# Attention and two channel mixers on one core: loads of both heads merged, and the load of grouped values moved from SyncE's queue to GpSimd's

## The chip, the cores and the metric

The kernel runs on one core of a Trainium2 chip. The metric is device time in microseconds (us) for one execution. Before the change three executions took 503.38, 504.46 and 505.86 us, so the median is 504.46 us. A core has a matrix engine (TensorE, PE), a vector engine (VectorE, DVE), a scalar engine (ScalarE, ACT), GpSimd (POOL) and SyncE (SP). Each runs its own instructions in order and they meet at semaphores. Loads from device memory go through 16 DMA engines.

## The reference

For batch 2, 8 heads, 768 positions and head dimension 64, every query attends to the keys less than 16 positions away and to 24 summaries, one per block of 32 positions: the maximum of the block's keys, with the mean of its values. Two channel mixers follow.

```python
k_sum = k.reshape(B, H, nb, 32, D).max(axis=3)
v_sum = v.reshape(B, H, nb, 32, D).mean(axis=3)
scores_l = where(|i - j| < 16, scale * q @ k.T, -1e9)
scores_s = scale * q @ k_sum.T + log(32)
a = softmax(concat([scores_l, scores_s], -1))
x = a @ concat([v, v_sum])                      # then heads side by side: (2, 768, 512)
h = relu(x.T @ w_tok1) @ w_tok2;  u = x + h.T   # mixing over positions
y = u + relu(u @ w_ch1) @ w_ch2                 # mixing over channels
# second mixer: xk, xr mix y with y shifted by one position
out = sigmoid(xr @ w_r) * (relu(xk @ w_k) ** 2 @ w_v)
```

## The kernel before

Attention works on pairs of heads: 16 (batch, head) rows make 8 pairs, p = 0 to 7. Pairs 0 to 5 are a loop of three turns with two pairs each (par is 0 or 1 and picks one of two buffers), pairs 6 and 7 stand behind it. A pair has three groups (r = 0, 1, 2) of four units, a unit being 64 queries of both heads. While pair p is computed, pair p+2 is prepared, with its own loads:

- kn and qn are the keys and queries as they lie in memory, turned by the PE (line 895), copied by ACT and DVE into kt and qbd.
- v8 holds the values of both heads in rows of 8 positions (96 rows, 2 heads, 512 values). POOL's `sum_values` adds them in three steps, v8 to v4 (line 436), v4 to v2 (438), v2 to v1 (441). The PE then sums groups of four rows of v1 into the 24 block means (`sum_vs`, line 918), ACT writes them to vsb, and SP spreads vsb over the twelve units of vw (`spread_vs`, line 321).
- vw holds the windows of values that the PE multiplies with the turned weights aT (line 998). For each head there are ten windows of 96 rows in the middle and one of 80 rows at each end.

No scheduler moves anything: every engine runs what is written, in that order. What matters here is the order of four of them within pair p.

**PE**, `pair`: for each r it turns the exponentials (line 976), forms scores of pair p+1 (928), and multiplies by the values (998). In r = 0 it turns kn of pair p+2 between scores and values, in r = 1 qn. In r = 2 `sum_vs(p + 2)` stands between scores and values, and it waits for v1 of pair p+2.

**POOL**, `pair`: `sum_values(p + 2)`, then the low part of a token-mixing weight (wt1L or wt2L, line 451), which waits for DVE's high part (733), then `split_x(p)` (line 457), which waits for the high part of the output of pair p itself (ACT, and DVE's line 724, after the last product of the pair and its normalisation). So POOL leaves pair p only after the PE has finished it.

**DVE**, after the values of r = 2: row sums (703), the weight's high part (733), the inverse (707), normalisation (716), high part of x (724).

**SP**, `pair`: spread vsb, four loads of kn and qn of pair p+2, a wait for `tree_step` and two loads of v8 of pair p+2, a wait until the PE has finished pair p-1 (`av_done`), six loads of vw of pair p+1, and one weight load into stg. v8 has one buffer; `tree_step` counts POOL's first two additions, so the load of pair p+2 may start once v4 of pair p+1 is there.

Ahead of the loop POOL fills constants (lines 400 to 431) and runs `sum_values(0)` and `sum_values(1)`. Semaphores that count loads go up by 16 for each.

Of the kernel before, what the change touches and what calls it, by code (L numbers as in the profile page):

```python
# [18 lines left out]
def build_program(nc, q, k, v, w_tok1, w_tok2, w_ch1, w_ch2, mu_k, mu_r, w_k, w_v, w_r, out):  # L19
    B, NH, S, D = q.shape  # L20
# [5 lines left out]
    SUMB, WIN = 32, 16  # L26
# [3 lines left out]
    UQ = 64  # L30
# [22 lines left out]
    with ctx:  # L53
# [159 lines left out]

        heads = "b h (t p j) d -> (b h) p t (j d)"
        q_rows = q.rearrange(heads, t=NB, j=2)
        k_rows = k.rearrange(heads, t=NB, j=2)
        v_rows8 = v.rearrange("b h (p j) d -> (b h) p (j d)", j=8)
        vt = v.tensor
# [4 lines left out]

        v_first = v_window(0, LOC - WIN, 1)
        v_mid = v_window(UQ - WIN, LOC, NU - 2)
        v_last = v_window(S - UQ - WIN, LOC - WIN, 1)
        w1_cols = w_ch1.rearrange("(k p) n -> p k n", p=P)
# [69 lines left out]
        def _(sp):  # L297
            def load_qk(p, par):
                for dst, src, loaded in ((kn, k_rows, ld_k), (qn, q_rows, ld_q)):
                    for h in range(2):  # L300
                        sp.dma_start(dst[par][:, h, :, :],  # L301
                                     src[bass.ds(2 * p + h, 1)].rearrange("o p t n -> (o p) t n")
                                     ).then_inc(loaded[par], 16)

            def load_vw(p, par):
                for h in range(2):
                    for dst, src in ((vw[par][WIN:LOC, 0:1, h, 0:D], v_first),
                                     (vw[par][0:LOC, 1:NU - 1, h, 0:D], v_mid),
                                     (vw[par][0:LOC - WIN, NU - 1:NU, h, 0:D], v_last)):
                        sp.dma_start(dst, src[bass.ds(2 * p + h, 1)].rearrange("o p t n -> (o p) t n")  # L310
                                     ).then_inc(ld_vw[par], 16)

            def load_v8(p):
                for h in range(2):
                    sp.dma_start(v8[:, h, :, :].rearrange("p j d -> p (j d)"),
                                 v_rows8[bass.ds(2 * p + h, 1)].rearrange("o p n -> (o p) n")
                                 ).then_inc(ld_v8, 16)

# [8 lines left out]
            load_qk(1, 1)  # L327
            load_v8(0)
            sp.wait_ge(init_pool, 2)
            load_vw(0, 0)  # L330
            with nc.allow_non_contiguous_dma(reason="two short vectors"):
                for n in range(2):
                    sp.dma_start(mu[:, n, :], mu_cols[n]).then_inc(ld_mu, 16)
            sp.wait_ge(tree_step, 1)
            load_v8(1)

            def pair(p, par, i=None):
                sp.wait_ge(qbank_read, 5 * p + 5)
                spread_vs(par)
                if i is not None:  # L340
                    sp.wait_ge(q_turned, 2 * p + 2)
                    sp.wait_ge(k_turned, 2 * p + 2)
                    load_qk(p + 2, par)
                    sp.wait_ge(tree_step, 2 * p + 3)
                    load_v8(p + 2)
                sp.wait_ge(av_done, 3 * p + 1)
                load_vw(p + 1, 1 - par)
                if i is not None:
                    sp.wait_ge(wl_done, p + 1)
                    src = t1_rows[:, bass.ds(2 * i, 2), :] if par == 0 else t2_rows[:, :, bass.ds(TOK * i, TOK)]  # L350
                    sp.dma_start(halves(stg[par][:, 0:512]), src).then_inc(ld_w[par], 16)
# [39 lines left out]
        def _(pool):  # L391
            steps = [0]

            def then(ins):
# [26 lines left out]
            for h in range(2):  # L421
# [9 lines left out]
                               pattern=[[-1, LOC]], channel_multiplier=0).then_inc(init_pool, 1)  # L431

            def sum_values(p):

                pool.wait_ge(ld_v8, 32 * p + 32)
                pool.tensor_tensor(v4[:, :, :, :], v8[:, :, 0:4, :], v8[:, :, 4:8, :], ALU.add).then_inc(tree_step, 1)
# [6 lines left out]
            def pair(p, par, i=None):  # L443
                if i is not None:
                    sum_values(p + 2)
                    pool.wait_ge(wh_done, p + 1)
# [12 lines left out]

            sum_values(0)  # L460
            sum_values(1)
            with pool.Fori(0, NP // 2 - 1) as i:
# [429 lines left out]
        def _(pe):  # L892
# [39 lines left out]
            pe.wait_ge(init_pool, 3)  # L932
            turn_k(0, 0, 32, None)
            turn_q(0, 0, 32, bT, False)
            pe.wait_ge(kt_written, 4)
            scores(0, 0, 0, 0, None)
            scores(0, 0, 1, 1, None)
            sum_vs(0, None)
            turn_k(1, 1, 32, 5)
            scores(0, 0, 2, 0, GU)  # L940
            turn_q(1, 1, 32)
            sum_vs(1, 7)
# [28 lines left out]
            def pair(p, par, prep):  # L971
                for r in range(NG):
# [7 lines left out]
                    if prep and r == 0:  # L980
                        turn_k(p + 2, par, 16 * (p - par) + 64, 5 * (p + 2))
                    if prep and r == 1:
                        turn_q(p + 2, par, 16 * (p - par) + 64)
                    if prep and r == NG - 1:
# [5 lines left out]
                    if r == 0:  # L990
                        pe.wait_ge(ld_vw[par], 48 * (p - par) + 96)
                        pe.wait_ge(ld_vs[par], 8 * (p - par) + 16)
# [152 lines left out]
```

## Time and profile before

| | |
|---|---|
| executions | 503.38, 504.46, 505.86 us; median 504.46 |
| span of the profiled execution | 501.4 us |
| PE busy over the span | 478.4 us (95%) |
| ACT busy / DVE busy / POOL busy | 191.6 / 221.7 / 114.6 us |
| instructions | 8399 |
| packets moved by DMA | 48657, 31.70 MB |

The profile is of one execution whose own total time is not given beside its span; the median of the executions is 3.1 us above that span. Busy time counts work on an engine, not waits. Attention fills the first 98 us; the rest is the mixers, in which the PE is nearly always busy. "SPq" or "POOLq" rows are an engine's queue at work on DMA issues or registers.

### The profile page before, as it was taken

How to read it: one execution, taken by the hardware profiler on the slowest of the kernel's cores; microseconds unless marked ns; L12 is line 12 of the kernel's file. 1: busy time of each engine (PE TensorE's matmuls, PEld its weight loads, DVE VectorE, ACT ScalarE, POOL GpSimd, SP SyncE). 2: the span in 40 equal slices, each digit the busy share in tenths (PEclk: the TensorE clock that was granted, in tenths of full speed). 3: DMA queues.
4: the chain of work that ended last, by engine and by line, in shares of the span. 5: the costliest groups of instructions: out<-in, count | busy, mean ns of one | idle time of the engine just before them, and what ended most of it. 6: DMA issues, size and time to landing. Idle time of an engine off the chain costs nothing.

```text
span 501.4 us, 8399 instructions
## 1 busy us (share of the span) xinstructions
PE 478.4 (95%) x2968; PEld 444.9 (89%) x2968; DVE 221.7 (44%) x575; ACT 191.6 (38%) x424; POOL 114.6 (23%) x98
## 2 busy tenths in 40 slices
PE   4798789998999999999999999999999999999996
PEld 4677678787999999999999999999889989989985
DVE  5598887499411141114111411456436355444521
ACT  3799887424211121112111211345455256353411
POOL 6364553285999000000000024300000000000000
PEclk9999999999999999999999999999999999999999
DMA  9999997144443100000000010000010001001001
GB/s 196 181 208 215 228 213 186 46 126 129 166 149 145 43 1 0 0 0 0 0 0 0 0 42 0 0 1 0 1 49 14 0 21 42 0 0 63 0 0 63
DMA packets 48657, 31.70 MB, mean 63 GB/s; under 512 B 21248, under 2 KB 42496, under 8 KB 48640
## 3 DMA queue, kind: packets, MB, share of 16 engines
q1 hardware_dynamic: 48640, 31.49, 26.4%
q8 instruction: 9, 0.15, 0.1%
q14 instruction: 8, 0.07, 0.1%
HBM read 27.14 MB, written 3.15 MB: 60 GB/s over the span
## 4 chain that ended last, share of the span: by engine, by line
PE 84%; SPq 5%; DMA 5%; ACT 2%; issue 2%; DVE 1%; POOL 0%; ACTq 0%; POOLq 0%
PE bank L946 26%; PE bank L947 26%; PE bank L948 26%; DMA kn<-in_k_dram 4%; SPq L301 2%; PE bank L998 1%; SPq L310 1%; DMA v<-in_v_dram 1%; PE bank L976 1%; ACT e_sb L518 1%; PE bank L1017 1%; ACT qbd L498 1%; PE bank L895 1%; SPq L321 1%; PE bank L928 1%
## 5 line engine op out<-in xcount | busy, mean ns | idle before, releaser
L845 DVE SCALAR_TENSOR_TENSOR rL<-bank,rH 128x384 fp32r<-128x384 f32 x48 | 26.7, 557 | 148.2 <-ACT rH L614 148.2
L614 ACT ACTIVATE rH<-bank 128x384 fp32r<-128x384 f32 x48 | 23.6, 492 | 163.1 <-PE bank L948 158.7
L946 PE MATMUL bank<-uH,W1H 128*128 128x384 f32 x192 | 64.8, 337 | 0.0
L947 PE MATMUL bank<-uL,W1H 128*128 128x384 f32 x192 | 64.6, 336 | 0.0
L948 PE MATMUL bank<-uH,W1L 128*128 128x384 f32 x192 | 64.4, 336 | 0.0
L947 PE MATMUL bank<-xkL,WkH 128*128 128x384 f32 x128 | 43.3, 338 | 0.0
L946 PE MATMUL bank<-xkH,WkH 128*128 128x384 f32 x128 | 43.1, 337 | 0.0
L948 PE MATMUL bank<-xkH,WkL 128*128 128x384 f32 x128 | 42.8, 335 | 0.0
L947 PEld LDWEIGHTS bank<-uL,W1H 128*128 128x128 f32 x192 | 36.1, 188 | 0.0
L948 PEld LDWEIGHTS bank<-uH,W1L 128*128 128x128 f32 x192 | 36.0, 188 | 0.0
L946 PEld LDWEIGHTS bank<-uH,W1H 128*128 128x128 f32 x192 | 36.0, 188 | 0.0
L482 POOL CAST W2aH<-stg 128x1024 fp32r<-128x1024 f32 x3 | 3.1, 1040 | 142.3 <-PE bank L948 142.3
L871 DVE SCALAR_TENSOR_TENSOR k<-bank,kr 128x384 f32<-128x384 f32 x32 | 17.8, 556 | 38.7 <-ACT kr L631 38.6
L948 PE MATMUL bank<-rH,W2aL 128*128 128x384 f32 x96 | 32.3, 336 | 0.0
L948 PE MATMUL bank<-rH,W2bL 128*128 128x384 f32 x96 | 32.3, 336 | 0.0
L946 PE MATMUL bank<-rH,W2bH 128*128 128x384 f32 x96 | 32.2, 335 | 0.0
L947 PE MATMUL bank<-rL,W2bH 128*128 128x384 f32 x96 | 32.2, 335 | 0.0
L946 PE MATMUL bank<-rH,W2aH 128*128 128x384 f32 x96 | 32.2, 335 | 0.0
L947 PE MATMUL bank<-rL,W2aH 128*128 128x384 f32 x96 | 32.2, 335 | 0.0
L631 ACT ACTIVATE kr<-bank 128x384 f32<-128x384 f32 x32 | 15.7, 489 | 43.1 <-PE bank L948 42.7
L518 ACT ACTIVATE e_sb<-s_sb,nmx 128x120 f32<-128x120 f32 x96 | 29.7, 382 | 3.3 <-DVE nmx L693 3.3
L928 PE MATMUL bank<-kw,qbd 128*128 128x120 f32 x192 | 27.6, 292 | 1.8 <-ACT qbd L498 1.6
(131 smaller groups left out, 1093.2 us busy)
## 6 DMA issues: line engine op xcount, KB each, us to landing
stg<-in_moe_w_ch_dram SPq DMA_DIRECT2D x12, 512.0 KB, 3.6
vw<-in_v_dram SPq DMA_DIRECT2D x16, 240.0 KB, 4.9
kn<-in_k_dram SPq DMA_DIRECT2D x16, 192.0 KB, 3.8
qn<-in_q_dram SPq DMA_DIRECT2D x16, 192.0 KB, 4.4
v<-in_v_dram SPq DMA_DIRECT2D x16, 192.0 KB, 5.1
out_dram<-o_sb SPq DMA_DIRECT2D x12, 256.0 KB, 2.0
stg<-in_moe_w_k_dram SPq DMA_DIRECT2D x4, 512.0 KB, 3.5
stg<-in_moe_w_v_dram SPq DMA_DIRECT2D x4, 512.0 KB, 3.4
```

Source lines behind the costliest of these rows:

```text
L301: sp.dma_start(dst[par][:, h, :, :], src[bass.ds(2 * p + h, 1)].rearrange("o p t n -> (o p) t n")).then_inc(loaded[par], 16)
L310: sp.dma_start(dst, src[bass.ds(2 * p + h, 1)].rearrange("o p t n -> (o p) t n")).then_inc(ld_vw[par], 16)
L321: sp.dma_start(vw[par][LOC:COLS, :, :, :].rearrange("p t h n -> p t (h n)"), vsb[par][:, :, :].rearrange("p h n -> p (h n)").unsqueeze(1) ...
L518: act.activation(e_sb[par][:, n, :], s_sb[r][:, n, :], ACT.Exp, bias=nmx[:, r, n:n + 1], scale=-1.0).then_inc(exp_done, 1)
L614: act.activation(rH[f % 2][:, :], bank[f % 2][:, 0:GR], ACT.Relu).then_inc(rh_done, 1)
L631: act.activation(kr[f % 2][:, :], bank[f % 2][:, 0:GR], ACT.Relu).then_inc(kr_done, 1)
L845: dve.scalar_tensor_tensor(out=rL[f % 2][:, :], in0=bank[f % 2][:, 0:GR], scalar=0.0, in1=rH[f % 2][:, :].bitcast(F32), op0=ALU.max, op1=A ...
L871: dve.scalar_tensor_tensor(out=k2[f % 2][:, :], in0=bank[f % 2][:, 0:GR], scalar=0.0, in1=kr[f % 2][:, :], op0=ALU.max, op1=ALU.mult).then ...
L928: ins = pe.matmul(bS[gp][:, COLS * n:COLS * n + COLS], qbd[par][:, t, :], kw[par][:, t, :], start=True, stop=True)
L946: pe.matmul(dst, wH, mH, start=start, stop=False, **more)
L947: pe.matmul(dst, wH, mL, start=False, stop=False, **more)
L948: return pe.matmul(dst, wL, mH, start=False, stop=stop, **more)
```

## The change

The loads of kn and of qn take both heads in one DMA each (six blocks of 128 values in place of three, twice). The end windows of vw take both heads in one DMA each, while the middle windows stay one per head. The load of v8 takes both heads in one DMA and is issued by POOL: for pair 0 as POOL's first instruction, for pair 1 between `sum_values(0)` and `sum_values(1)`, and for pair p+2 at the beginning of POOL's `pair`, just before `sum_values(p + 2)`. The semaphore counts follow. Bytes, packets and the arithmetic are the same. With spread and weight load, SP issues eight DMAs for a pair where it issued fourteen; POOL issues one.

```diff
             def load_qk(p, par):
                 for dst, src, loaded in ((kn, k_rows, ld_k), (qn, q_rows, ld_q)):
-                    for h in range(2):
-                        sp.dma_start(dst[par][:, h, :, :],
-                                     src[bass.ds(2 * p + h, 1)].rearrange("o p t n -> (o p) t n")
-                                     ).then_inc(loaded[par], 16)
+                    sp.dma_start(dst[par][:, :, :, :].rearrange("p h t n -> p (h t) n"),
+                                 src[:, bass.ds(2 * NB * p, 2 * NB), :]).then_inc(loaded[par], 16)
 
             def load_vw(p, par):
                 for h in range(2):
-                    for dst, src in ((vw[par][WIN:LOC, 0:1, h, 0:D], v_first),
-                                     (vw[par][0:LOC, 1:NU - 1, h, 0:D], v_mid),
-                                     (vw[par][0:LOC - WIN, NU - 1:NU, h, 0:D], v_last)):
-                        sp.dma_start(dst, src[bass.ds(2 * p + h, 1)].rearrange("o p t n -> (o p) t n")
-                                     ).then_inc(ld_vw[par], 16)
-
-            def load_v8(p):
-                for h in range(2):
-                    sp.dma_start(v8[:, h, :, :].rearrange("p j d -> p (j d)"),
-                                 v_rows8[bass.ds(2 * p + h, 1)].rearrange("o p n -> (o p) n")
-                                 ).then_inc(ld_v8, 16)
+                    sp.dma_start(vw[par][0:LOC, 1:NU - 1, h, 0:D],
+                                 v_mid[bass.ds(2 * p + h, 1)].rearrange("o p t n -> (o p) t n")
+                                 ).then_inc(ld_vw[par], 16)
+                for dst, src in ((vw[par][WIN:LOC, 0, :, 0:D], v_first),
+                                 (vw[par][0:LOC - WIN, NU - 1, :, 0:D], v_last)):
+                    sp.dma_start(dst, src[:, bass.ds(2 * p, 2), :]).then_inc(ld_vw[par], 16)
...
                     load_qk(p + 2, par)
-                    sp.wait_ge(tree_step, 2 * p + 3)
-                    load_v8(p + 2)
                 sp.wait_ge(av_done, 3 * p + 1)
...
         def _(pool):
             steps = [0]
+            pool.dma_start(v8[:, :, :, :].rearrange("p h j d -> p h (j d)"),
+                           v_rows8[:, 0:2, :]).then_inc(ld_v8, 16)
...
+            def load_v8(p):
+                pool.dma_start(v8[:, :, :, :].rearrange("p h j d -> p h (j d)"),
+                               v_rows8[:, bass.ds(2 * p, 2), :]).then_inc(ld_v8, 16)
+
             def sum_values(p):
 
-                pool.wait_ge(ld_v8, 32 * p + 32)
+                pool.wait_ge(ld_v8, 16 * p + 16)
...
             def pair(p, par, i=None):
                 if i is not None:
+                    pool.wait_ge(tree_step, 2 * p + 3)
+                    load_v8(p + 2)
                     sum_values(p + 2)
...
             sum_values(0)
+            pool.wait_ge(tree_step, 1)
+            load_v8(1)
             sum_values(1)
```

What POOL's queue holds in the loop, from one `split_x` (xL) to the additions of the next pair, first before, then with the change (each with the line numbers of its own kernel; v_79 is v8, v_80 is v4, v_81 is v2, v_82 is v1; ISA and REGISTER_ALU are address arithmetic and waits).

```order
L457 TENSOR_TENSOR xL<-u,xH 128x768
L435 ISA
L436 TENSOR_TENSOR v_80<-v_79 96x512 [waits ld_v8]
L437 ISA
L438 TENSOR_TENSOR v_81<-v_80 96x256 [waits tree_step]
```

```order
L456 TENSOR_TENSOR xL<-u,xH 128x768
L442 ISA
L427 ISA [waits tree_step]
L427 DMA v_79<-in_v_dram 96x2x512
L432 ISA
L433 TENSOR_TENSOR v_80<-v_79 96x512 [waits ld_v8]
```

The load now stands between the xL of one pair and the addition that reads what it loads.

SP's queue in the loop, from the wait for the finished pair to the last load of vw, first before, then with the change, where the row of qn just ahead is shown too (vw_73 is the buffer of odd pairs).

```order
L310 ISA [waits av_done]
L310 DMA vw_73<-in_v_dram 80x64
L310 ISA
L310 DMA vw_73<-in_v_dram 96x10x64
L310 ISA
L310 DMA vw_73<-in_v_dram 80x64
L310 ISA
L310 DMA vw_73<-in_v_dram 80x64
L310 ISA
L310 DMA vw_73<-in_v_dram 96x10x64
L310 ISA
L310 DMA vw_73<-in_v_dram 80x64
```

```order
L303 DMA qn_75<-in_q_dram 128x6x128
L337 ISA
L308 ISA [waits av_done]
L308 DMA vw_73<-in_v_dram 96x10x64
L308 ISA
L308 DMA vw_73<-in_v_dram 96x10x64
L313 REGISTER_ALU
L313 DMA vw_73<-in_v_dram 80x2x64
L313 ISA
L313 DMA vw_73<-in_v_dram 80x2x64
```

Two end loads are gone from this stretch, the two middle ones come first, and no load of v8 stands ahead of the wait.

## Rows read from the trace of the kernel before

**Rows 1.** The page: chain that ended last, by engine and by line.

```profile
PE 84%; SPq 5%; DMA 5%; ACT 2%; issue 2%; DVE 1%; POOL 0%; ACTq 0%; POOLq 0%
PE bank L946 26%; PE bank L947 26%; PE bank L948 26%; DMA kn<-in_k_dram 4%; SPq L301 2%; PE bank L998 1%; SPq L310 1%; DMA v<-in_v_dram 1%; PE bank L976 1%; ACT e_sb L518 1%; PE bank L1017 1%; ACT qbd L498 1%; PE bank L895 1%; SPq L321 1%; PE bank L928 1%
```

**Rows 2.** Busy time by stretch: start:end and length, engines, clock, DMA share, GB/s.

```profile
core 0: us, PE busy (x) PEld busy (x) DVE busy (x) ACT busy (x) POOL busy (x), PEclk, DMA share, GB/s
13.00:16.00 3.00, 1.51 (x7) 0.89 (x7) 0.90 (x8) 1.97 (x8) 1.09 (x2) 1.00 0.71 143
29.51:78.87 49.36, 42.81 (x491) 36.29 (x492) 42.03 (x201) 44.64 (x122) 27.80 (x25) 1.00 1.18 214
```

**Rows 3.** Timeline of SP's queue: start us, us, what; first loads, then one pair.

```profile
12.87 0.80 SPq L315 DMA_DIRECT2D v<-in_v_dram  x2
...
18.86 0.82 SPq L315 DMA_DIRECT2D v<-in_v_dram  x2
...
55.77 0.84 SPq L321 DMA_DIRECT2D vw<-vsb  x1
56.99 1.13 SPq L301 DMA_DIRECT2D kn<-in_k_dram  x2
58.22 0.97 SPq L301 DMA_DIRECT2D qn<-in_q_dram  x2
59.37 0.82 SPq L315 DMA_DIRECT2D v<-in_v_dram  x2
60.49 3.59 SPq L310 DMA_DIRECT2D vw<-in_v_dram  x6
64.27 0.39 SPq L351 DMA_DIRECT2D stg<-in_moe_w_tok_dram  x1
```

**Rows 4.** Timeline of the PE: last product of pairs 0, 3 and 5, and what precedes it.

```profile
14.22 0.62 PE L918 MATMUL bank<-v,sel 96*24 96x128 f32 x2 [1.04 <-POOL v L441]
...
28.77 0.74 PE L998 MATMUL bank<-vw,aT 120*64 120x65 f32 x16
...
58.59 0.40 PE L918 MATMUL bank<-v,sel 96*24 96x128 f32 x2 [0.80 <-POOL v L441]
58.91 0.74 PE L998 MATMUL bank<-vw,aT 120*64 120x65 f32 x16
...
78.14 0.73 PE L998 MATMUL bank<-vw,aT 120*64 120x65 f32 x16
```

**Rows 5.** Timeline of POOL: additions of pairs 0 to 2, then the turn of pair 3 to 4.

```profile
8.90 0.27 POOL L430 TENSOR_SCALAR_AFFINE_SELECT mask<-mask 128x96 f32<-128x96 f32 x1
11.57 1.27 POOL L436 TENSOR_TENSOR v<-v 96x512 f32<-96x512 f32 x1 [2.40 <-DMA v<-in_v_dram]
...
16.28 1.27 POOL L436 TENSOR_TENSOR v<-v 96x512 f32<-96x512 f32 x1 [2.11 <-DMA v<-in_v_dram]
...
24.89 1.27 POOL L436 TENSOR_TENSOR v<-v 96x512 f32<-96x512 f32 x1 [6.01 <-DMA v<-in_v_dram]
...
57.54 0.92 POOL L441 TENSOR_TENSOR v<-v 96x128 f32<-96x128 f32 x1 [0.25 <-POOL v L438]
60.44 1.27 POOL L451 TENSOR_TENSOR wt2L<-stg,wt2H 128x512 f32 x1 [1.98 <-DVE wt2H L733]
62.38 1.69 POOL L457 TENSOR_TENSOR xL<-u,xH  x1 [0.67 <-DVE xH L724]
64.56 1.27 POOL L436 TENSOR_TENSOR v<-v 96x512 f32<-96x512 f32 x1 [0.50 <-DMA v<-in_v_dram]
...
66.80 0.46 POOL L441 TENSOR_TENSOR v<-v 96x128 f32<-96x128 f32 x1 [0.16 <-POOL v L438]
```

**Rows 6.** Who waited for whom, all of the execution: us, times, longest.

```profile
PE bank L895 <- DMA kn<-in_k_dram: 8.5, 6, 4.4
```

**Rows 7.** Timeline of DVE: the high part of x beside POOL's work, and alone.

```profile
61.05 0.80 DVE L724 CAST xH<-u  x1 [0.16 <-DVE u L716]
...
89.02 0.29 DVE L724 CAST xH<-u 128x256 fp32r<-128x256 f32 x1
```

**Rows 8.** One line each (315, 441): ns min/median/max; us to landing min/median/max.

```profile
L315 SPq DMA_DIRECT2D v<-in_v_dram x16: 329/367/484, 5.0 to 68.9; - x16
DMA to landing us min/median/max: 2.8/5.1/6.2
...
L441 POOL TENSOR_TENSOR v<-v x8: 451/454/917, 13.7 to 77.0; 96x128 f32<-96x128 f32 x8
```

More of the change, by code:

```diff
@@ L211, in build_program @@
         ld_out = sem("ld_out")
[L214 to L217, printed above, removed]
+        blocks = "b h (t p j) d -> p (b h t) (j d)"
+        q_rows = q.rearrange(blocks, t=NB, j=2)
+        k_rows = k.rearrange(blocks, t=NB, j=2)
+        v_rows8 = v.rearrange("b h (p j) d -> p (b h) (j d)", j=8)
         vt = v.tensor
@@ L222, in v_window, with v_end @@
             return bass.AP(vt, first_row * D, [[S * D, B * NH], [D, rows], [UQ * D, units], [1, D]])
-        v_first = v_window(0, LOC - WIN, 1)
+        def v_end(first_row):
+            return bass.AP(vt, first_row * D, [[D, LOC - WIN], [S * D, B * NH], [1, D]])
         v_mid = v_window(UQ - WIN, LOC, NU - 2)
-        v_last = v_window(S - UQ - WIN, LOC - WIN, 1)
+        v_first, v_last = v_end(0), v_end(S - UQ - WIN)
         w1_cols = w_ch1.rearrange("(k p) n -> p k n", p=P)
@@ L327, in _ @@
             load_qk(1, 1)
-            load_v8(0)
             sp.wait_ge(init_pool, 2)
@@ L333, in _ @@
                     sp.dma_start(mu[:, n, :], mu_cols[n]).then_inc(ld_mu, 16)
-            sp.wait_ge(tree_step, 1)
-            load_v8(1)
             def pair(p, par, i=None):
@@ L932, in _ @@
             pe.wait_ge(init_pool, 3)
-            turn_k(0, 0, 32, None)
-            turn_q(0, 0, 32, bT, False)
+            turn_k(0, 0, 16, None)
+            turn_q(0, 0, 16, bT, False)
             pe.wait_ge(kt_written, 4)
@@ L938, in _ @@
             sum_vs(0, None)
-            turn_k(1, 1, 32, 5)
+            turn_k(1, 1, 16, 5)
             scores(0, 0, 2, 0, GU)
-            turn_q(1, 1, 32)
+            turn_q(1, 1, 16)
             sum_vs(1, 7)
@@ L980, in pair @@
                     if prep and r == 0:
-                        turn_k(p + 2, par, 16 * (p - par) + 64, 5 * (p + 2))
+                        turn_k(p + 2, par, 8 * (p - par) + 32, 5 * (p + 2))
                     if prep and r == 1:
-                        turn_q(p + 2, par, 16 * (p - par) + 64)
+                        turn_q(p + 2, par, 8 * (p - par) + 32)
                     if prep and r == NG - 1:
@@ L990, in pair @@
                     if r == 0:
-                        pe.wait_ge(ld_vw[par], 48 * (p - par) + 96)
+                        pe.wait_ge(ld_vw[par], 32 * (p - par) + 64)
                         pe.wait_ge(ld_vs[par], 8 * (p - par) + 16)
```

## Prediction

> **What bounds the kernel now.** I read the page's chain of what ended last first: 84% of the span is PE, and of the rest nearly all is SP's queue and the DMA of kn [rows 1]. The chain in order of time puts both into attention, the first 98 us; behind it the mixers keep the PE busy and start from wherever attention ends. So the question is only how the pairs of attention move.
>
> In a pair's steady state I take as its mark the end of the last product of r = 2, T(p+1), when pair p is done. T1 is 28.77 + 0.74 = 29.51, T4 is 58.91 + 0.74 = 59.65 and T6 is 78.14 + 0.73 = 78.87 [rows 4]. Five pairs (1 to 5) take 49.36 us, 9.87 us each. In that stretch ACT is busy 44.64 us, 8.93 us a pair, PE 42.81 and POOL 27.80 [rows 2]: ACT is near its limit, POOL has nearly half its time free. What costs the last microsecond is SP: its queue works almost without a break through fourteen issues, from 55.77 to 64.66 [rows 3], and kn is issued so late that the PE waits for it. That wait is 8.5 us in six times, of which the first, 4.4 us, is the start [rows 6]; about 4.1 us is left in the loop, 0.8 us a pair.
>
> Second, DMA itself: its busy share averages 1.18 in the stretch (packets overlap) at 214 GB/s [rows 2]. The bytes don't change, so fewer issues cannot make the data much faster.
>
> **The parts of the change.** *Merged kn, qn and end windows.* Per pair SP loses two issues of kn and qn (about half of 1.13 and 0.97), two small ones of vw, and the two of v8 (0.82 together): by 0.4 to 0.5 us each with the registers between them, some 2.5 to 3 us [rows 3]. By itself this takes the wait for kn away. Its worth has a floor, ACT's 8.93 us: at most 9.87 - 8.93 = 0.94 us a pair, 4.7 us in five pairs.
>
> *The load of v8 on POOL.* Here the order of POOL's queue decides. Before, SP issued v8 of pair p+2 while POOL was still in the pair before, so that the data landed about when POOL arrived: of the whole landing POOL saw 0.50 us in the turn shown [rows 5]. After, POOL issues the load itself when it has left `split_x`, and then waits for all of it with nothing between. `split_x(p-1)` needs pair p-1 finished, and the PE needs v1 of pair p+2 before it can finish pair p. That closes a ring with the load in it, and I sum it from T4, the pair whose DVE was free when the product ended:
>
> - From T to the end of xL: 62.38 + 1.69 - 59.65 = 4.42 us (DVE's sums, the weight's high part, normalisation, high x, and POOL's low weight are in it) [rows 4, 5].
> - POOL's registers before the load: between 0 and the 0.50 us gap to the addition that follows; I take 0.10 [rows 5].
> - The load, from the start of its issue to the first addition: L, below.
> - The three additions: 66.80 + 0.46 - 64.56 = 2.70 us [rows 5].
> - From v1 to the next T: v1 ends at 57.54 + 0.92 = 58.46, T4 is 59.65: 1.19 us [rows 4, 5].
>
> The sum is 8.41 + L. It is longer than the present 9.87 as soon as L is over 1.46 us.
>
> **The size of L.** POOL issues no DMA in this trace, so L is bounded from both sides by SP's loads of v8. The shortest landing of one half is 2.8 us [rows 8]. For both halves with little other traffic: issued from 12.87, POOL starts at 16.28, 3.41 us; share of DMA in that stretch 0.71 [rows 2, 3, 5]. One merged issue in place of two saves about 0.4: 3.0 us is the lower end. With a full queue ahead: issued from 18.86, POOL starts at 24.89, 6.03 us, the upper end [rows 3, 5]. The new case lies nearer the lower: the same bytes are spread over a longer pair (1.18 x 9.87 / 12.5 = 0.93 of share), and the load no longer stands behind kn and qn in their queue, but shares the engines with vw, the weight and the next kn. Issuing on POOL may cost from SP's 0.37 us [rows 8] to that of an addition, 1.27 us [rows 5]. I take 3.0 + 0.5 for the issue + 0.6 for traffic = 4.1 us.
>
> By itself, and not used in the sum: the Trainium skill, page "DMA: Bandwidth & Descriptors", section "Anatomy of one DMA", puts a GpSimd-issued DMA at about 2.0 us plus bytes over 436 GB/s; for these 0.39 MB that is an estimate of 2.9 us, and the ring 11.3 us. No row here shows a POOL DMA; the measured 3.4 us on SP is already longer, and the sum goes by that. The same page, "Rules for kernel authors", says that spreading issues over engines saves only the sequencer's issue time; that is the part worth at most 4.7 us above.
>
> **The sum.** A pair takes 8.41 + 4.1 = 12.5 us, 2.64 us more than 9.87. It holds for pairs 1 to 5, five times: +13.2 us. The gain from the merged loads is not added, since the ring through POOL is then longer than the one through SP, and ACT, PE and kn all wait in its shade. Pair 0 is not in the ring: no `split_x` stands before its load. POOL finishes v1 of pair 1 near where it did, at 16.28 + 2.70 = 19.0, and v1 of pair 2 even with L = 6 at 19.0 + 6 + 2.7 = 27.7, before the last product of pair 0 begins at 28.77 [rows 4, 5]. Pairs 6 and 7 load no v8.
>
> Start: v8 of pair 0 lands at about 5 instead of 11.57, so POOL adds from about 9.2 + 0.4 to 1.3 (its constants end at 9.17 and come later by the issue) [rows 5]. The PE waited 1.04 us for it at 14.22 [rows 4]. Most of that is gained, but v1 of pair 1 now comes after a load that is issued only at about 12.5 + 0.5, so it is not earlier than before. I take 0.5 us of gain; bounds 1.0 of gain and 0.9 of loss (the late constants delay the first transposes).
>
> In the profiled execution: 501.4 + 13.2 - 0.5 = 514.1 us of span. With the 3.1 us between span and median, **517 us**.
>
> **Rivals.** *The load slips out under xL.* POOL's queue could hand the load over while its engine is still at xL; then 1.69 us of the ring goes, and it is 6.7 + L. This is the case that can end on the other side: with L = 4.1 it is 10.8, +4.8 us, 509; from L = 3.1 downwards no pair is longer than now, and the time is 504 or, with the start's gain, just below. For it: the queue already works registers ahead of the engine. Against: a load that GpSimd itself makes should wait its turn there. 11%, of which 5% ends at or below 504.
>
> *The load is quick, 3.0 to 3.6 us.* Then +7.9 to +10.8, less 0.5: 512 to 515. 16%.
>
> *The load is slow, 5 to 6.6 us,* because it stands beside full queues or its issue is held up. POOL and DVE hold each other up here: DVE's cast of x takes 0.80 us beside POOL's work, 0.29 alone [rows 7], and POOL's last addition 454 ns in the middle, 917 at most [rows 8]. An issue that is doubled so costs 0.5 to 1.3 us more. L = 5.4 gives +19.7 - 0.5 = 524. 16%. The Trainium skill, page "SBUF — State Buffer", section on bandwidth pools, has a GpSimd DMA of 620 ns that took 3100 ns under a VectorE copy, since its descriptors could not be written; by that, 2.5 us more a pair in the worst case, an estimate of 529. The rows show the lock on arithmetic, not yet on a DMA.
>
> *The data is there anyway, and SP's gain shows:* this needs L under 1.46 us, and no landing is under 2.8 [rows 8]. It would give 504.5 - 4.7 = 500. 2%.
>
> **How the numbers follow.** My forecast, L between 3.6 and 5, has 55%, and gives 514 to 521. Beside it 16% quick, 16% slow, 11% under xL, 2% gain. The range of 8 in 10 leaves out the ones under xL and the slowest: 510 to 526. A measurement of this kernel can tell about 0.5% (2.5 us) from no change. Faster by more than that: 3%; within: 4%; slower: 93%.
>
> **What would show it.** In the changed profile T(p+1) - T(p) should be 12 to 13 us for pairs 1 to 5; POOL's first addition should wait 3.5 to 4.5 us for the DMA of v in each; the PE's longest waits should be at the sum of values (918 before) for POOL, and none for kn. SP's queue should show gaps before vw, waiting for the PE. The prediction is wrong if POOL's wait for v is short, if kn still holds the PE, or if T6 comes before 82.

## The result, and the profile after

The changed kernel takes **530.10 us** (median of four executions, 529.35 to 530.84) against 503.92 us for the kernel before (four, 502.51 to 505.86): a ratio of 1.053 [1.051, 1.056], 26 us slower. (The brackets hold a 95% interval.) The forecast was 517 us with a range of 510 to 526. The direction and the ring through GpSimd were right, the size was not: 13.1 us are missing. Below, two single slower executions, one of e8 at 952.20 us, for which no reason is known, and one of e9 at 508.96, are left out of medians and ratios.

The page of the profile after, which answers to [rows 1] (busy time, then the chain that ended last, by engine and by line):

```profile
PE 484.2 (92%) x2968; PEld 450.7 (85%) x2968; DVE 224.6 (42%) x575; ACT 193.5 (37%) x424; POOL 119.5 (23%) x106
...
PE 80%; issue 9%; POOL 6%; DVE 3%; DMA 1%; POOLq 1%; ACT 0%; DVEq 0%
PE bank L947 25%; PE bank L948 25%; PE bank L949 25%; POOL v L433 2%; PE bank L999 2%; POOL v L435 1%; PE bank L1018 1%; DMA v<-in_v_dram 1%; DVE xH L725 1%; POOL v L427 1%; POOL v L438 1%; PE bank L977 1%; PE bank L919 1%; PE bank L929 1%; DVE u L717 0%
```

SP's queue and the DMA of kn, 5% and 4% before, are gone. In their place stand POOL's additions, its load of v, and DVE's line 725: the links of the ring that the prediction drew.

The same marks T as in [rows 4], on the PE, with the turn from pair 1 to pair 2 between them:

```profile
30.13 0.73 PE L999 MATMUL bank<-vw,aT 120*64 120x65 f32 x16
...
45.27 0.62 PE L919 MATMUL bank<-v,sel 96*24 96x128 f32 x2 [7.02 <-POOL v L438]
45.82 1.19 PE L999 MATMUL bank<-vw,aT 120*64 120x65 f32 x16
46.94 1.11 PE L977 MATMUL bank<-ident,e_sb 128*120 128x128 f32 x4
47.84 1.78 PE L929 MATMUL bank<-kw,qbd 128*128 128x120 f32 x8
...
105.77 0.74 PE L999 MATMUL bank<-vw,aT 120*64 120x65 f32 x16
```

T1 is 30.13 + 0.73 = 30.86 and T6 is 105.77 + 0.74 = 106.51: five pairs take 75.65 us, 15.13 each, where they took 9.87. The PE stands still for 7.02 us before it can sum the values of pair 3, waiting for POOL's third addition, v1.

POOL in the same turn, to be held beside [rows 5]:

```profile
34.11 1.68 POOL L456 TENSOR_TENSOR xL<-u,xH  x1 [1.09 <-DVE xH L725]
35.74 0.65 POOL L427 DMA_DIRECT2D v<-in_v_dram  x1
42.49 1.25 POOL L433 TENSOR_TENSOR v<-v 96x512 f32<-96x512 f32 x1 [6.09 <-DMA v<-in_v_dram]
43.81 0.72 POOL L435 TENSOR_TENSOR v<-v 96x256 f32<-96x256 f32 x1
44.69 0.45 POOL L438 TENSOR_TENSOR v<-v 96x128 f32<-96x128 f32 x1 [0.16 <-POOL v L435]
...
49.74 1.68 POOL L456 TENSOR_TENSOR xL<-u,xH  x1 [0.67 <-DVE xH L725]
51.36 0.65 POOL L427 DMA_DIRECT2D v<-in_v_dram  x1
...
98.45 0.65 POOL L427 DMA_DIRECT2D v<-in_v_dram  x1
102.26 1.25 POOL L433 TENSOR_TENSOR v<-v 96x512 f32<-96x512 f32 x1 [3.16 <-DMA v<-in_v_dram]
```

The load starts within 0.05 us of the end of xL (34.11 + 1.68 = 35.79), and nothing stands between it and the addition that needs it. L, from 35.74 to 42.49, is 6.75 us here; the five loads of the ring give 6.75, 6.89, 6.10, 7.35 and, for the last, from 98.45 to 102.26, only 3.81. What SP's queue does just then:

```profile
34.13 0.84 SPq L317 DMA_DIRECT2D vw<-vsb  x1
35.36 0.41 SPq L303 DMA_DIRECT2D kn<-in_k_dram  x1
35.86 0.70 SPq L303 DMA_DIRECT2D qn<-in_q_dram  x1
47.21 0.95 SPq L308 DMA_DIRECT2D vw<-in_v_dram  x2
```

kn goes out 0.38 us ahead of v8 and qn 0.12 us behind it, 384 KB each. In the last turn of the ring no kn or qn is left to load, and L is 3.81.

Who waited for whom in attention, in us, times, and the longest:

```profile
POOL v L433 <- DMA v<-in_v_dram: 37.1, 7, 6.7
...
PE bank L919 <- POOL v L438: 27.7, 7, 7.0
```

There is no wait for kn in the loop any more. Busy time by stretch (columns as in [rows 2]):

```profile
38.00:45.00 7.00, 0.25 (x3) 0.06 (x1) 1.96 (x11) 1.82 (x6) 2.28 (x3) 0.82 0.60 132
45.00:50.00 5.00, 4.73 (x35) 4.22 (x36) 1.94 (x6) 2.73 (x8) 1.68 (x3) 0.56 0.41 80
...
61.00:66.00 5.00, 4.96 (x34) 4.46 (x35) 2.10 (x6) 2.73 (x8) 1.54 (x2) 0.50 0.49 86
30.86:106.51 75.65, 49.75 (x492) 43.37 (x492) 43.48 (x200) 46.04 (x121) 30.25 (x30) 0.84 0.67 134
```

From 38 to 45 us the PE works 0.25 of 7 us. Then it starts again at a granted clock of 0.56 and, a pair later, 0.50: about the lower of its two levels, 1.2 GHz in place of 2.4. The sixteen products of line 999 take 1.19 us instead of 0.73.

The ring's terms in us, as the prediction named them (means of the five turns):

| term | predicted | measured |
|---|---|---|
| T to the end of xL | 4.42 | 4.60 |
| before the load | 0.10 | -0.05 |
| L | 4.1 | 6.18 |
| three additions | 2.70 | 2.74 |
| v1 to the next T | 1.19 | 1.67 |
| a pair | 12.5 | 15.13 |

Five pairs: 5 x (15.13 - 12.5) = 13.1 us over what the sum gave them. T1 came 30.86 - 29.51 = 1.35 later where 0.5 of gain was forecast, 1.85 more. The rest behind T6 takes 529.1 - 106.51 = 422.6 us, as before (501.4 - 78.87 = 422.5). So 514.1 + 13.1 + 1.85 = 529.1 us: the span, with nothing left over. Against the median the miss is 13.1 us (the same number as the ring's by chance) and not 529.1 - 514.1 = 15.0, since the 3.1 us that the prediction put between span and median were too many: each of the four executions took 1.7 to 1.9 us more than its own span, the profiled one 530.84 against 529.1.

### The profile page after: what moved, and what is told of

Same layout as the page of the kernel before. It is cut to its first block, busy times and chain, and to the rows that moved or that the text cites. A ratio compares the mean times of both kernels' runs of the same rounds, so it can differ in the third digit from the quotient of the medians.

```text
span 529.1 us, 8325 instructions
## 1 busy us (share of the span) xinstructions
PE 484.2 (92%) x2968; PEld 450.7 (85%) x2968; DVE 224.6 (42%) x575; ACT 193.5 (37%) x424; POOL 119.5 (23%) x106
## 4 chain that ended last, share of the span: by engine, by line
PE 80%; issue 9%; POOL 6%; DVE 3%; DMA 1%; POOLq 1%; ACT 0%; DVEq 0%
PE bank L947 25%; PE bank L948 25%; PE bank L949 25%; POOL v L433 2%; PE bank L999 2%; POOL v L435 1%; PE bank L1018 1%; DMA v<-in_v_dram 1%; DVE xH L725 1%; POOL v L427 1%; POOL v L438 1%; PE bank L977 1%; PE bank L919 1%; PE bank L929 1%; DVE u L717 0%
## 5 line engine op out<-in xcount | busy, mean ns | idle before, releaser
L929 PE MATMUL bank<-kw,qbd 128*128 128x120 f32 x192 | 30.1, 311 | 1.7 <-ACT qbd L499 1.7
```

What stands on the lines that cost most here:

```text
L929: ins = pe.matmul(bS[gp][:, COLS * n:COLS * n + COLS], qbd[par][:, t, :], kw[par][:, t, :], start=True, stop=True)
```

## The experiments

Each ran beside the kernel before on the same chip. "Pair" is (T6 - T1)/5 of its profile, in us, and L is as above, in the order of the turns. A profile shows one execution: that of e1, e2, e4, e8, e10 and e11 is the fastest of its run, that of the changed kernel, e5 and e7 the slowest, so a difference of some tenths of a us between pairs of two profiles says little. The questions: is it the place of the load in POOL's order or the merging; why is L 6 to 7 us and not 4; what makes v1 to T longer; and can the good parts be kept.

### e1: everything merged, the load of v8 left with SP

The change without its move: v8 merged too, issued by SP where it stood.

```diff
                     load_qk(p + 2, par)
+                    sp.wait_ge(tree_step, 2 * p + 3)
+                    load_v8(p + 2)
...
                 if i is not None:
-                    pool.wait_ge(tree_step, 2 * p + 3)
-                    load_v8(p + 2)
                     sum_values(p + 2)
```

> The changed kernel with the load of v8 given back to SyncE, where it stood before (behind kn and qn, one merged DMA); all merged loads stay. Theory 'order' (the loss is the place of the v8 load in POOL's queue, the whole landing in a ring that closes once a pair): the ring is gone, the pairs fall from 15.1 us to between 9.0 and 9.9, and the time is 499 to 504 us. Rival 'merge' (the merged kn and qn loads themselves land late, 5.9 and 7.4 us in place of 3.8 and 4.4, and slow everything): the time stays at least 5 us above the kernel before, 509 or more.

Measured: 502.90 us against 503.05, 1.000 [0.997, 1.004]; pair 9.67. So all of the loss is in the move of v8, and the merging by itself is worth nothing that can be measured here, though SP issues nine DMAs a pair instead of fourteen. The PE still waits for kn between T1 and T6, 2.8 us in three times where it was 4.1 in five. v8, issued at 36.70, is first read at 43.10: its L, 6.40 us, is as long as in the changed kernel, but POOL's other work lies beside it and leaves 1.23 us of waiting. SP's queue:

```profile
37.65 1.97 SPq L308 DMA_DIRECT2D vw<-in_v_dram  x2
39.81 3.35 SPq L313 DMA_DIRECT2D vw<-in_v_dram  x2
...
49.38 4.22 SPq L313 DMA_DIRECT2D vw<-in_v_dram  x2
```

Two small end loads hold SP for 3.35 us (0.93 us for the same two in the changed kernel, where SP has waited for the PE first), and the median landing of vw's middle loads is 6.4 us in place of 4.9. The bytes moved per second are the same (210 GB/s from 31 to 77 us, 214 before). I read this as SP reaching vw sooner and standing there behind bytes not yet moved; the rows show the longer issues, not what they wait for.

### e2: only v8 moved to GpSimd

The kernel before with nothing merged but v8, and that on POOL as in the change.

```diff
                     load_qk(p + 2, par)
-                    sp.wait_ge(tree_step, 2 * p + 3)
-                    load_v8(p + 2)
...
                 if i is not None:
+                    pool.wait_ge(tree_step, 2 * p + 3)
+                    load_v8(p + 2)
                     sum_values(p + 2)
```

> The kernel before with only the load of v8 moved to POOL as in the change; kn, qn and vw keep their fourteen-per-pair form less v8. Theory 'order': the ring is whole, pairs of 14.5 to 15.5 us, 526 to 533 us. Rival 'merge': the landing of v8 falls back towards 3.5 to 4.5 us since kn and qn come in smaller pieces, pairs of 12 to 13 us, 514 to 520 us.

Measured: 527.51 us, 1.048 [1.042, 1.054]; pair 13.88; L 5.54, 4.92, 5.00, 5.33, 4.58. The move alone makes nearly the whole loss. But its pairs are shorter than 15.13, which I had not expected. In its first turn v8 goes out at 36.87 and kn only at 37.44, since SP has more to issue before it; in the changed kernel kn is ahead of v8. Merging brought kn forward into the load of v8. This is a reading of one profile each: the intervals of the two times overlap, and the medians lie 2.6 us apart, 0.5 a pair, not 1.25.

### e3: GpSimd's load issued one pair ahead

The load stays on POOL, but the one for the next pair goes out as soon as v8 has been read.

```diff
                 pool.wait_ge(tree_step, 2 * p + 1)
+                if more:
+                    load_v8(p + 1)
...
                 if i is not None:
-                    pool.wait_ge(tree_step, 2 * p + 3)
-                    load_v8(p + 2)
-                    sum_values(p + 2)
+                    sum_values(p + 2, more)
```

> The changed kernel, GpSimd still issues v8, but the load for the next pair goes out right behind the addition that frees the buffer (v8 to v4) and not at the beginning of the next pair; POOL's last two pairs of the loop are written out for it. Theory 'order': POOL finds the data there, no wait for v over 1 us in the loop, pairs of 9.0 to 10 us, 499 to 505 us. Rival 'issuer' (a load issued by GpSimd is slow or disturbs in itself, by its 0.65 us on POOL and by a landing of 6.6 us): the pairs stay above 11 us, 510 us or more.

Measured: 506.00 us, 1.006 [1.003, 1.008]; pair 10.26. POOL waits for v once in these five pairs, for 0.44 us. It is not that GpSimd issues, it is where in its order it does. Where the 0.6% that is left comes from is not shown. In the four turns with a load, and a wait before it, between the additions, these now take 3.5 to 4.3 us from first to last where they took 2.7; but the PE waits for v1 only once in these pairs, 1.6 us, and for kn three times, 4.1 us together.

### e4: SP issues v8 as late as POOL did

```diff
                     load_qk(p + 2, par)
+                    sp.wait_ge(xl_done, p + 1)
+                    load_v8(p + 2)
                 sp.wait_ge(av_done, 3 * p + 1)
...
+            sp.wait_ge(tree_step, 3)
             with sp.Fori(0, NP // 2 - 1) as i:
```

and POOL loads nothing.

> The changed kernel with v8 issued by SyncE (merged, hardware queue), but only after POOL's xL of the pair before is done, so as late as POOL issued it; it stands behind kn and qn in SyncE's queue. One wait for the second v4 is put ahead of the loop, under 1 us once. Theory 'order': the ring is there with another issuer, a load of 5.5 to 7 us, pairs of 14 to 15.5 us, 523 to 532 us. Rival 'issuer': hardware-issued, the load lands in 3.5 to 4.5 us from the release and the time is 513 to 519 us.

Measured: 522.04 us, 1.036 [1.031, 1.042]; pair 13.02. The two views agree: SP's queue, then POOL.

```profile
35.30 0.34 SPq L316 DMA_DIRECT2D v<-in_v_dram  x1
```

```profile
38.81 1.85 POOL L441 TENSOR_TENSOR v<-v 96x512 f32<-96x512 f32 x1 [3.69 <-DMA v<-in_v_dram]
```

L is 3.51, 3.72, 4.07, 3.81 and 3.52. The place alone, with no GpSimd DMA in the kernel at all, turns the 9.67 us a pair of e1 into 13.0. It is not a clean test of the issuer: here kn and qn had gone out 6 us or more before v8. vw's loads go out from 35.92, 0.62 us behind v8 and in the same queue, and L stays near the 3.81 us of the changed kernel's last turn.

### e5: kn and qn held until v8 has landed

The changed kernel, with one wait more on SP.

```diff
                     sp.wait_ge(k_turned, 2 * p + 2)
+                    sp.wait_ge(ld_v8, 16 * p + 32)
                     load_qk(p + 2, par)
```

> The changed kernel, with one wait more: SyncE issues kn and qn of pair p+2 only when v8 of pair p+1 has landed, so that GpSimd's load has the DMA engines nearly to itself. Theory 'beside' (of the 6.75 us of the load about 3 come from kn and qn, merged and asked for in the same half microsecond): the load takes 3.8 to 4.5 us as it did for pair 7, pairs fall from 15.1 to 12.2 to 13.2 us and the time to 514 to 520 us. Rival 'issuer' (GpSimd's descriptors are written slowly while DVE copies and adds): the load stays at 6 us or more and the time at 526 or more.

Measured: 523.36 us, 1.040 [1.034, 1.045]; pair 13.86; L 5.44, 4.55, 4.61, 4.86, 4.56. POOL's rows, and SP's kn behind them:

```profile
35.99 0.66 POOL L428 DMA_DIRECT2D v<-in_v_dram  x1
41.43 1.25 POOL L434 TENSOR_TENSOR v<-v 96x512 f32<-96x512 f32 x1 [4.78 <-DMA v<-in_v_dram]
```

```profile
41.54 0.40 SPq L303 DMA_DIRECT2D kn<-in_k_dram  x1
```

In the first four turns, those with kn and qn, L falls from a mean of 6.77 to 4.87 us: 1.9 us of L are these two loads beside it. A kernel with one more wait is 7 us quicker than the changed one. I had expected 514 to 520, with L at 3.8 to 4.5. The rest is not kn and qn: the last turn, which has neither in any version, takes 4.56 here, 3.81 in the changed kernel and 3.73 to 4.58 over all versions that load late in GpSimd's or ScalarE's queue; why it varies is open. And v1 to T is still 1.86 or 1.87 in three of the turns.

### e6: v8 through ScalarE's queue, at the same moment

```diff
                     if prep and r == 0:
+                        act.wait_ge(xl_done, p + 1)
+                        load_v8(p + 2)
                         turn_out_k(p + 2, 2 * p + 4)
```

and none on POOL; ACT also loads the first two.

> The changed kernel with v8 issued by ScalarE, whose queue is a hardware one of its own, at the same moment as GpSimd did it (after xL of the pair before) and so again beside kn and qn. ScalarE stands still for up to 1.7 us a pair until xL is done, which the long pairs hide. Theory 'beside': the load takes 5.5 to 7 us whoever issues it, pairs of 14 to 15.5 us, 522 to 531 us. Rival 'issuer': it takes 3.5 to 4.8 us, pairs of 12 to 13.3 us, 513 to 519 us.

Measured: 534.21 us, 1.063 [1.057, 1.068]; pair 14.98. ACT's row, then POOL's:

```profile
37.76 0.34 ACTq L510 DMA_DIRECT2D v<-in_v_dram  x1
```

```profile
43.05 1.71 POOL L431 TENSOR_TENSOR v<-v 96x512 f32<-96x512 f32 x1 [5.49 <-DMA v<-in_v_dram]
```

L is 5.29, 6.56, 6.37, 6.58, and 3.73 in the last turn: the pattern of the changed kernel with another issuer. With kn and qn beside it the mean is 6.20 against 6.77, without them 3.73 against 3.81. Through GpSimd the load costs 0.57 us more in the mean, of which 0.3 is the issue (0.65 and 0.34 us); the turns of the two overlap. The traffic is the main cause. The whole is slower than the changed kernel, but not in the ring, whose pairs are no longer though ACT now stands waiting for xL (2.92 us at 38.29): T1 is 33.00, 2.1 us later, since the loads for pairs 1 and 2 go out at 14.63 and 22.88 in place of 12.91 and 20.01, and the part behind T6 takes 1.6 us more, for a reason that was not looked for.

The Trainium skill, page "DMA: Bandwidth & Descriptors", section "Issuing engines are not separate DMA queues", says that DMAs of ScalarE, SyncE and GpSimd run on the same 16 engines and interleave. These rows agree: 6.2 and 6.8 us beside kn and qn, 3.7 and 3.8 alone.

### e7: products that keep the PE busy

Sixteen products of constants, written to a bank that is overwritten afterwards, stand before the wait for v1. They add work and take none away.

```diff
                     if prep and r == NG - 1:
+                        pe.wait_ge(qbank_read, 5 * (p + 2) + 2)
+                        for fill in range(16):
+                            pe.matmul(bQ[0:NSUM, 0:P], sel[:, :], ident[0:96, :], start=True, stop=True)
                         sum_vs(p + 2, 5 * (p + 2) + 2)
```

> The changed kernel with 16 extra products of constants on the PE, in pairs 0 to 5, just before the product that waits for v1; they land in the bank that this product then overwrites, and fill about 2 to 4 us of its 4 to 7 us of waiting. Theory 'clock' (the PE's waits lowered its granted clock, and the slower products that follow v1 cost 0.7 to 1 us of each ring): the granted clock is nearer 1.00 in the pairs, and the time falls by 3 to 5 us, to 525 to 527. Rival: the slower products are hidden in the wait and the time stays within 1 us of the changed kernel.

Measured: 531.62 us, 1.055 [1.049, 1.061]; pair 14.96. The total did not fall, but two turns show the clock apart. The PE's rows with what is left of the gap, then the stretches behind them:

```profile
48.05 0.62 PE L919 MATMUL bank<-v,sel 96*24 96x128 f32 x2 [3.30 <-POOL v L438]
...
63.64 0.40 PE L919 MATMUL bank<-v,sel 96*24 96x128 f32 x2 [0.87 <-POOL v L438]
```

```profile
48.00:52.00 4.00, 3.95 (x29) 3.43 (x30) 1.85 (x5) 2.12 (x7) 1.26 (x1) 0.50 0.22 51
63.00:67.00 4.00, 3.36 (x43) 2.92 (x45) 1.89 (x6) 2.67 (x8) 1.72 (x2) 1.00 0.28 65
```

Behind 3.30 us of waiting the clock is 0.50 and v1 to T takes 1.80 us; behind 0.87 us it is 1.00 and v1 to T takes 1.11. So the 0.7 us of that term is the clock. How long the last wait was does not settle the clock: the next turn has 0.58 and 1.80 us behind a wait of only 2.06. In e2 the sixteen products are still quick behind a longer one:

```profile
72.59 0.39 PE L917 MATMUL bank<-v,sel 96*24 96x128 f32 x2 [3.56 <-POOL v L436]
72.92 0.74 PE L997 MATMUL bank<-vw,aT 120*64 120x65 f32 x16
```

In pair 0 the filler outlasts the wait (v1 to T is 3.82 there), so T1 is 33.77, 2.9 us later than in the changed kernel, of which the five pairs give back 0.9.

### e8 and e9: versions meant to keep the gain

e8 is e3 with the load behind v1 instead of between the additions:

```diff
                 pool.tensor_tensor(v1[:, :, :], v2[:, :, 0, :], v2[:, :, 1, :], ALU.add).then_inc(v1_ready, 1)
+                if more:
+                    load_v8(p + 1)
```

> As the kernel with GpSimd's load one pair ahead, but the load goes out behind the last addition (v1), so that its 0.65 us and the wait ahead of it no longer stand between v4 and v1. Theory 'order': v1 comes about 0.9 us sooner in each pair, the loads start 2 us later but still land before POOL comes back; 502 to 505 us. Rival: the later load is late again, waits for v of over 1 us in the loop, 507 us or more.

Measured: 504.80 us, 1.003 [1.000, 1.005]; pair 9.23 in its profile, whose own execution took 501.79, the fastest of nine.

```profile
39.07 0.65 POOL L427 DMA_DIRECT2D v<-in_v_dram  x1 [0.18 <-issue]
...
44.84 1.28 POOL L433 TENSOR_TENSOR v<-v 96x512 f32<-96x512 f32 x1
```

The load takes nearly as long as in the changed kernel (median landing 6.2 us, there 6.6), but the addition shows no wait: the weight's low part and xL lie between. Five pairs at 9.23 are 3.2 us quicker than at 9.87, the start is 1.6 later (T1 31.13), and the median shows none of the rest.

e9 gives the first two loads back to SP, with a semaphore of their own:

```diff
             load_qk(1, 1)
+            load_v8_first(0)
             sp.wait_ge(init_pool, 2)
...
+            sp.wait_ge(tree_step, 1)
+            load_v8_first(1)
```

> Merged loads; v8 of pairs 0 and 1 issued by SyncE (a semaphore of their own), v8 of pairs 2 to 7 by GpSimd one pair ahead, behind v1. Theory: the start of the kernel with all loads on SyncE (T1 near 28) and the pairs of the kernel with the load ahead behind v1 (9.2 us) add up: T6 near 74 to 75.5 in place of 78.9, 498.5 to 501 us. Rival: a quicker start or a shorter pair only meets the DMA engines' own limit, T6 at 77 to 79 and 502 to 505 us.

Measured: 503.25 us over eleven executions (500.38 to 506.29) against 503.76, 1.000 [0.997, 1.003]. In its profile T1 is 29.85, but the pairs take 10.29 us: kn holds the PE for 2.11 us at 72.45. The two gains did not add up.

### e10: the changed kernel with SP's start

The first diff of e9 on the changed kernel, whose loop stays as it is.

> The changed kernel with only v8 of pairs 0 and 1 given back to SyncE; in the loop GpSimd loads as in the change. Theory 'start' (GpSimd's first load, issued at 1.5 us ahead of its constants, delays the PE's first turns and with them all of pair 0): T1 comes at 28 to 29 in place of 30.9, the pairs stay at 15 us, 526.5 to 528.5 us. Rival: pair 0 waits for something else, T1 stays at 30 or more and the time at 529.5 to 531.

Measured: 530.04 us, 1.056 [1.052, 1.059]; T1 29.29, pair 14.92. The start in the profile is 1.57 us earlier than 30.86, near the 28 to 29 expected, and that profile's execution took 528.15. The other five took 529.5 to 534.9, so the median shows no gain and the 526.5 to 528.5 us expected are missed.

### e11: e9 with kn, qn and vw unmerged

```diff
-                    sp.dma_start(dst[par][:, :, :, :].rearrange("p h t n -> p (h t) n"),
-                                 src[:, bass.ds(2 * NB * p, 2 * NB), :]).then_inc(loaded[par], 16)
+                    for h in range(2):
+                        sp.dma_start(dst[par][:, h, :, :],
+                                     src[bass.ds(2 * p + h, 1)].rearrange("o p t n -> (o p) t n")
+                                     ).then_inc(loaded[par], 16)
```

> As the kernel with the start on SyncE and the load ahead, but kn, qn and vw are loaded in their fourteen-per-pair form (less the two of v8). If SyncE's issue time is what merging saves, its pairs are 0.4 to 0.8 us longer and the time 2 to 4 us above that kernel; if the DMA engines' backlog is the limit by then, the two agree within 1.5 us.

Measured: 506.07 us, 1.006 [1.004, 1.008]; 2.8 us above e9, with which it shares the runs of before, and the two intervals do not overlap. With v8 out of SP's queue, merging the others is worth about 0.6%. The profiles don't show where: T1 is 28.98 and the pair 10.29, the same as in e9. No version tried is quicker than the kernel before beyond doubt.

## Why the prediction was wrong

**What bounds the kernel: right.** Only the pairs of attention and the start moved; behind T6 nothing changed (422.6 and 422.5 us).

**The worth of merged issues: right in its bound, wrong in its reason.** I bounded it by ACT's 8.93 us a pair, 4.7 us in all. e1 shows about none, and "By itself this takes the wait for kn away" failed there: 2.8 of 4.1 us stayed. That the wait is gone in the changed kernel is no success of the merging, since there the pairs are longer and e1, with the same merged loads, keeps it. In e1 the issue time came back at vw's end loads; the remark that fewer issues can't make the data much faster fits it, but was not tested by itself. The 2.8 us between e9 and e11 lie within the bound.

**The ring: right.** e1 and e2 put the loss on the move, e4 on its place with no GpSimd DMA at all, and e3 and e8 take it away with the load still on POOL.

**Which term failed: L, 6.18 instead of 4.1.** It is 5 x 2.08 = 10.4 of the 13.1 us in the ring: the mechanism was right and this term was mis-sized. The step was "I take 3.0 + 0.5 for the issue + 0.6 for traffic". I had spread the same bytes evenly over a longer pair, a share of 0.93, and argued that v8 no longer stands behind kn and qn in their queue. But a turn of the ring releases them together: SP spreads vsb and issues kn and qn at 35.36 and 35.86, and POOL issues v8 at 35.74. The mean share over five pairs did fall, to 0.67, and said nothing about the microseconds in which L lies. e5 moves kn and qn away and takes 1.9 us off L; the last turn, which has neither, takes 3.81; e6 has nearly the same lengths with another issuer. In e7 and e10, whose loads in the loop stand as in the change, L is 5.76 to 7.56 us in the turns with kn and qn and 3.80 and 4.13 in the last. The neighbours of a load at the moment of its issue, in all queues, were to be read from the order, and I had only read the queue it left.

The kernel before could have told this too. There POOL waits for v8 in each of the five turns, so the time from SP's issue to the first addition is the length of that load behind the same bytes of kn and qn. In the turn of [rows 3] and [rows 5] it is 64.56 - 59.37 = 5.19 us, and the longest is 6.76, from SP's queue to POOL:

```profile
48.45 0.82 SPq L315 DMA_DIRECT2D v<-in_v_dram  x2
```

```profile
55.21 1.27 POOL L436 TENSOR_TENSOR v<-v 96x512 f32<-96x512 f32 x1 [1.64 <-DMA v<-in_v_dram]
```

The five give 5.57, 5.69, 6.76, 5.19 and 6.27, a mean of 5.90. With that for L the prediction's own sum comes to 14.3 us a pair and, as an estimate, 526 us. The upper bound of 6.03, taken from the start, was too low already there, and four of the ring's five turns passed it.

**The slow rival was the case,** by the first of its two reasons, full queues. Its other reason, GpSimd and VectorE holding each other up, adds little if anything: the issue takes 0.65 us in the loop, 0.3 more than through ACT, and L 0.57 more. (The quick rival's "+7.9 to +10.8" comes to +7.7 to +10.7 by its own sum; nothing hangs on it.) By the rival's own sum, with L at 6.18, a pair would be 8.41 + 6.18 = 14.6 and the time 528. The Trainium skill, page "SBUF — State Buffer", section "SBUF: two separate sides", says that a load issued through ScalarE or SyncE runs at full speed beside VectorE's copy. e6 is such a load and takes 6.20 us beside kn and qn, so the lock can hardly account for more than the 0.57 us between it and 6.77.

**v1 to T, 1.67 instead of 1.19.** It is 5 x 0.48 = 2.4 us. I took this term from a PE that had hardly waited [rows 4] and put it behind a wait of several us without asking what the wait does to the engine. In three of the five turns it is 1.86 or 1.87: the clock of 0.50 to 0.56 behind the gaps. e7 has both values in one kernel. In the other two turns it is 1.57 and 1.19. The clock's price is paid only where the PE is on the ring; lines 977 and 929 are slow too (1.11 and 1.78 us), but T to xL stays near 4.4 to 4.6 us, since that way leads through DVE and POOL.

**T to xL, +0.18.** In the first turn it is 4.93, in the others 4.41 to 4.63. I had summed it from T4; before the change it was 4.42 to 4.94, so T4 was the shortest. The other two terms, the registers (-0.15) and the additions (+0.04), are near nothing; with them the five differences come to 2.63 a pair.

**The start, +1.35 instead of -0.5.** The rows of POOL at the start, and the PE's first turn:

```profile
1.52 0.80 POOL L384 DMA_DIRECT2D v<-in_v_dram  x1 [0.87 <-POOLq L1133]
...
10.38 1.26 POOL L433 TENSOR_TENSOR v<-v 96x512 f32<-96x512 f32 x1
...
12.91 0.69 POOL L427 DMA_DIRECT2D v<-in_v_dram  x1
17.04 1.26 POOL L433 TENSOR_TENSOR v<-v 96x512 f32<-96x512 f32 x1 [3.44 <-DMA v<-in_v_dram]
...
20.01 0.66 POOL L427 DMA_DIRECT2D v<-in_v_dram  x1
26.68 1.26 POOL L433 TENSOR_TENSOR v<-v 96x512 f32<-96x512 f32 x1 [6.01 <-DMA v<-in_v_dram]
...
28.90 0.77 POOL L438 TENSOR_TENSOR v<-v 96x128 f32<-96x128 f32 x1 [0.16 <-POOL v L435]
```

```profile
5.15 1.54 PE L896 MATMUL bank<-ident,kn 128*128 128x128 f32 x6 [5.15 <-POOL sel L408]
```

v8 of pair 0 is there early, as forecast, but POOL's constants end at 10.15 + 0.27 = 10.42, 1.25 later than before, and hide it. The PE's first product too begins at 5.15, behind POOL's constants, where it began at 4.38. Then my sentence that v1 of pair 2 ends by 27.7, before it is needed, failed: v1 of pair 1 ends at 20.03 and not 19.0, the load takes 6.67 and not 6, and the additions 2.99. It ends at 28.90 + 0.77 = 29.67, and T1 follows 1.19 behind. So pair 0 is tied to the loads after all. e10 gives the start back in its profile; its executions don't show it, and what takes it back there is open.

**What stays open.** How the 13.0 us of e4 and the 15.13 part into neighbours and clock to a tenth: each experiment moves more than one of them. L alone is 3.73 there against 6.18, which is more than the difference. What sets the PE's clock behind a wait, beyond that it was low behind most long ones. Why L without kn and qn varies from 3.73 to 4.58. And why e8's pairs of 9.23 us and e10's earlier start do not show in the medians; both profiles are of the fastest execution, and one each is too few to say.

## What to carry to other kernels

When a load moves to another engine, write down what stands between its issue and its first use in the new queue; if nothing does, and that engine's last instruction waits for the step the load feeds, the whole landing becomes part of the period, whoever issues it. Price the landing by what the other queues release at the same event, not by a mean share: in the changed kernel 3.8 us without kn and qn and 6.1 to 7.4 beside these two loads of the same size. If the old queue already loaded it beside the same neighbours, its length there, from issue to first use, is the nearest row. Fewer DMA issues need not make a kernel quicker (e1: 1.000), and a long wait on the PE can make the work behind it slower (0.7 us between two turns of e7).

## What the runs showed of the hardware

- The PE's granted clock in the 4 or 5 us behind a wait was 0.56 after 7.02 us, 0.50 after 5.40 and 0.50 after 3.30, where sixteen products took 1.19 us, and 1.00 after 0.87. The length of the last wait alone did not decide: after 3.56 us in e2 sixteen products took 0.74 us, and after 2.06 us in e7 the clock was 0.58.
- A load of 384 KB without kn and qn beside it took 3.81 us through GpSimd, 3.73 through ScalarE, and 3.51 to 4.07 through SyncE with vw's loads 0.62 us or so behind it in the same queue. With kn and qn issued through SyncE within 0.5 us of it, it took 6.77 through GpSimd and 6.20 through ScalarE, means of four.
- An issue of v8 held GpSimd for 0.65 or 0.66 us in the changed kernel's loop and 0.80 at its start, up to 0.91 in e8; ScalarE for 0.32 to 0.46 in e6; and SyncE for 0.34 in the loop of e4. In none of the ring's turns did the load start more than 0.06 us ahead of the end of xL.
- SyncE's own issues can grow: two small loads of vw held it for 3.35 us in e1, behind kn, qn, v8 and two more loads issued in the 5 us before, and 0.93 in the changed kernel.
